# Probabilities times values per head in six spread slots, mirrored query order kept through the feed-forward, accumulators opened by transposes

## The reference

```
mask   = bucket(q @ proj) == bucket(k @ proj)          # 6 sign bits
attn   = softmax(where(mask, q @ k.T / 8, -1e9))       # 768 x 768 for each of 16 heads
x      = attn @ v, heads side by side                   # 2 x 768 x 512
u      = x + real(fft(fft(x, axis=seq), axis=feature))
ch     = relu(normalise(u) @ w_ch1) @ w_ch2             # 512 -> 2048 -> 512
x2     = u + ch
out    = (sigmoid(conv5(x2)) * (x2 @ w_val)) @ w_out
```

## Time and profile before

| | |
|---|---|
| median of the runs (3) | 663.28 us |
| the profiled execution | 663.62 us |
| its span (first to last instruction) | 661.8 us |
| PE busy / PEld busy | 634.2 us (96%) / 508.4 us (77%) |
| DVE, ACT, POOL busy | 353.8, 317.0, 245.4 us |
| chain that ended last: PE, DVE | 84%, 8% |
| granted TensorE clock | full in all of the 40 slices |

### The profile page before, as it was taken

One profiled execution on the slowest core, in us unless ns is written; L12 is line 12 of the kernel. 1 busy time (PEld: TensorE's weight loads), 2 busy tenths in 40 slices (PEclk: granted clock), 3 DMA queues, 4 the chain that ended last, 5 costly groups with the idle time before them and its releaser, 6 DMA issues.

```text
span 661.8 us, 11290 instructions
## 1 busy us (share of the span) xinstructions
PE 634.2 (96%) x3810; PEld 508.4 (77%) x3810; DVE 353.8 (53%) x585; ACT 317.0 (48%) x606; POOL 245.4 (37%) x201
## 2 busy tenths in 40 slices
PE   2999999999999999889999999999999999999998
PEld 1667676767666675888888888889888888888786
DVE  2978786968787785987211111115433333329920
ACT  2877776868686765364322222224333333255242
POOL 6643333333252440845333222235544444313140
PEclk9999999999999999999999999999999999999999
DMA  5922231314241000100122222431212222000102
GB/s 127 247 77 72 72 95 48 95 48 108 59 119 57 15 25 1 49 0 1 33 65 63 63 63 63 141 115 33 63 63 63 63 63 63 16 1 1 64 32 95
DMA packets 34263, 42.08 MB, mean 64 GB/s; under 512 B 3521, under 2 KB 22209, under 8 KB 34241
## 3 DMA queue, kind: packets, MB, share of 16 engines
q1 hardware_dynamic: 32512, 37.77, 19.7%
q0 software_dynamic: 1728, 4.02, 2.3%
HBM read 38.63 MB, written 3.15 MB: 63 GB/s over the span
## 4 chain that ended last, share of the span: by engine, by line
PE 84%; DVE 8%; issue 3%; POOL 2%; ACT 1%; DMA 1%; SPq 0%; DVEq 0%; ACTq 0%
PE banks L1516 20%; PE banks L1504 20%; PE banks L1319 10%; PE banks L1302 10%; PE banks L1366 7%; PE banks L1595 4%; PE banks L1611 4%; DVE row_min L970 2%; PE banks L1258 2%; PE banks L1439 2%; PE banks L1491 1%; DVE probT L342 1%; DVE k_b L963 1%; PE banks L1342 1%; POOL row_sums_and_differences L540 1%
## 5 line engine op out<-in xcount | busy, mean ns | idle before, releaser
L1165 DVE SCALAR_TENSOR_TENSOR h_lo<-banks,h_hi 128x512 fp32r<-128x512 f32 x64 | 35.5, 558 | 186.4 <-ACT h_hi L826 186.4
L970 DVE TENSOR_REDUCE row_min<-banks 128x1 f32<-128x768 f32 x96 | 91.3, 956 | 44.3 <-PE banks L1302 43.8
L677 ACT ACTIVATE prob<-banks,row_min 128x768 f32<-128x768 f32 x96 | 87.0, 906 | 30.1 <-DVE row_min L970 30.1
L1504 PE MATMUL banks<-unT_hi,w_hi 128*128 128x512 f32 (+1 forms) x256 | 86.5, 338 | 0.0
L1504 PE MATMUL banks<-unT_hi,w_lo 128*128 128x512 f32 (+1 forms) x256 | 86.3, 337 | 0.0
L1504 PE MATMUL banks<-unT_lo,w_hi 128*128 128x512 f32 (+1 forms) x256 | 86.2, 337 | 0.0
L1366 PE MATMUL banks<-ident,prob 128*128 128x128 f32 x576 | 79.7, 274 | 2.2 <-DVE probT L342 1.2
L563 POOL TENSOR_TENSOR w_lo<-w_stage,w_hi 128x512 fp32r<-128x512 f32 x32 | 45.1, 1411 | 83.2 <-ACT w_hi L742 83.2
L1366 PEld LDWEIGHTS banks<-ident,prob 128*128 128x128 f32 x576 | 67.2, 140 | 10.2 <-ACT probT L342 2.6
L501 POOL TENSOR_TENSOR k_b<-k_raw,k_a 64x768 fp32r<-64x768 f32 x16 | 29.2, 1823 | 123.2 <-ACT k_a L660 123.2
L1319 PE MATMUL banks<-probT,v_in 128*64 128x384 f32 x384 | 72.3, 498 | 0.7 <-ACT outT L687 0.7
(11 more groups left out here) (149 smaller groups left out, 1204.1 us busy)
## 6 DMA issues: line engine op xcount, KB each, us to landing
w_stage<-in_moe_w_ch SPq DMA_DIRECT2D x64, 256.0 KB, 2.8
q_raw<-in_q SPq DMA_DIRECT2D x32, 192.0 KB, 3.3
k_raw<-in_k SPq DMA_DIRECT2D x32, 192.0 KB, 3.6
v_in<-in_v SPq DMA_DIRECT2D x16, 192.0 KB, 2.4
out<-y_out SPq DMA_DIRECT2D x12, 256.0 KB, 2.0
seq_tables_sb<-in_dft POOLq DMA_DIRECT2D x6, 386.0 KB, 3.6
wvo_stage<-in_moe_w_val SPq DMA_DIRECT2D x1, 1024.0 KB, 5.4
wvo_stage<-in_moe_w_out SPq DMA_DIRECT2D x1, 1024.0 KB, 7.9
```

The costliest lines, as they stand in the source:

```text
L677: act.activation(prob[s % 2][:, :, :], s_tile(s), ACT.Exp, bias=row_min[:, s:s + 1], scale=-1.0, accum_out=row_sum[:, s:s + 1]).then_inc(e ...
L970: dve.tensor_reduce(row_min[:, s:s + 1], s_tile(s), AX.XY, ALU.min).then_inc(min_ready, 1)
L1165: dve.scalar_tensor_tensor(out=h_lo[:, slot, at:at + size], in0=h_bank[c], scalar=0.0, in1=h_hi[:, slot, at:at + size].bitcast(F32), op0=A ...
L1504: op = pe.matmul(h_bank[c], w_[:, slot, kb, :], x_[:, kb, at:at + size], start=(kb == 0 and m == 0), stop=(kb == KB - 1 and m == 2))
```

## The change

1. **Probabilities times values.** A group of products is now one head h with all 768 queries: the query half g = 0 in partitions 0 to 63 of bank 7, g = 1 in 64 to 127. There are still 24 matmuls a pair, in six groups of four, but the groups stand in slots 9, 11 (of the same pair), 1, 3, 5, 7 (of the next). `copy_outT` moves from slots 1 and 4 to 2 and 8, task O from slots 3 and 6 to 5 and 11, B from slots 1 and 7 to 0 and 6; C0 and C1 keep slots 2, 8 and 4, 10. The row sums are inverted per head, `write_x` writes 64 columns of six tiles instead of 128 columns of three. Since products now reach back further, pair 1 is written out and the loop runs over pairs 2 to 6.
2. **Row order.** `un_hi` and `un_lo` keep the folded order; `reverse` and `natural` are gone. `take_x2` restores the natural order while it drains, with one more instruction per block d (four instead of three, one of them a single column).
3. **Opening the accumulators.** `open_acc` issues one PE transpose for each of six tiles and each d: 24 a batch instead of 32 matmuls.
4. **Loads.** The values of each head have a semaphore and a load of their own; head 1's waits until the products of head 1 of the pair before are done.

```
-        PREPARE = {1: ["B"], 2: ["C0"], 4: ["C1"], 7: ["B"], 8: ["C0"], 10: ["C1"]}
+        PREPARE = {0: ["B"], 2: ["C0"], 4: ["C1"], 6: ["B"], 8: ["C0"], 10: ["C1"]}
-        OUT_SLOT = {3: 0, 6: 1}
+        OUT_SLOT = {5: 0, 11: 1}
-        PV_SLOTS = {11: (0, 0), 0: (0, 1), 1: (0, 2), 2: (1, 0), 3: (1, 1), 4: (1, 2)}
+        PV_SLOTS = {9: (0, 0, 0), 11: (0, 0, 1), 1: (1, 0, 2), 3: (1, 1, 0), 5: (1, 1, 1), 7: (1, 1, 2)}
...
-            def load_v(i):
-                need(sp, pv_done, 2 * i)
-                for h in range(2):
-                    sp.dma_start(v_in[:, h, :, :], v_v[2 * i + h]).then_inc(v_loaded, 16)
+            def load_v(i, h):
+                need(sp, pv_done, 2 * i + (h - 1) if not isinstance(i, int) or i else 0)
+                sp.dma_start(v_in[:, h, :, :], v_v[2 * i + h]).then_inc(v_loaded[h], 16)
...
-                    if s == 1 and not (isinstance(i, int) and i == 0):
+                    if s == 2 and not (isinstance(i, int) and i == 0):
                         copy_outT(i, 0)
-                    if s == 4 and not (isinstance(i, int) and i == 0):
+                    if s == 8 and not (isinstance(i, int) and i == 0):
                         copy_outT(i, 1)
...
-                    act.copy(half[:, 0:C0 - HALF], PS[:, d, HALF:C0]).then_inc(x2_by_act, 1)
-                    act.copy(half[:, C0 - HALF:HALF], acc(d, 1)).then_inc(x2_by_act, 1)
+                    act.copy(half[:, 0:1], PS[:, d, HALF:HALF + 1]).then_inc(x2_by_act, 1)
+                    act.copy(half[:, C1 + 1:HALF], PS[:, d, C0 - 1:HALF:-1]).then_inc(x2_by_act, 1)
+                    act.copy(half[:, C1:0:-1], acc(d, 1)).then_inc(x2_by_act, 1)
...
-                for kt in (2 * part, 2 * part + 1):
-                    for h in range(2):
-                        op = pe.matmul(PS[h * D:(h + 1) * D, 7, 0:HALF], v_in[:, h, kt, :],
+                for kt in range(T // PV_PARTS * part, T // PV_PARTS * (part + 1)):
+                    for g in range(2):
+                        op = pe.matmul(PS[g * D:(g + 1) * D, 7, 0:HALF], v_in[:, h, kt, :],
                                        probT[h][:, kt, g * HALF:(g + 1) * HALF], start=(kt == 0), stop=(kt == T - 1))
...
+                tiles = (range(C0 // P), range(C0 // P, T))[c]
+                for t in tiles:
+                    at = t * P - c * C0
+                    pe.matmul(acc(d, c)[:, at:at + P], X[:, b, t, d * P:(d + 1) * P], ident[:, :], is_transpose=True,
+                              start=(t == tiles[0] and (c == 0 or d % 2 == 0)), stop=False, skip_group_check=True)
```

More of the change, by code:

```diff
@@ L335, in drain_prob @@
             wait_filled(eng, i, use)
-            if h == 0 and qt % HT == 0:
-                need(eng, pv_done, pair_ * 2 + (qt // HT - 1))
+            if qt == 0:
+                need(eng, pv_done, pair_ * 2 + (h - 1))
             half = int(task[1])
@@ L428, in _ @@
             load_qk(0, 1)
-            load_v(0)
+            load_v(0, 0)
+            load_v(0, 1)
             load_qk(1, 0)
@@ L481, in _ @@
             pool.memset(ident[:, :], 0.0).then_inc(consts_ready, 1)
[L482 to L485, removed]
+            pool.wait_ge(consts_ready, 6)
             pool.affine_select(out=ident[:, :], in_=ident[:, :], compare_op=ALU.not_equal, fill=1.0,
@@ L732, in _ @@
             pair(0, 0)
-            with act.Fori(1, NP - 1) as i:
+            pair(1, 0)
+            with act.Fori(2, NP - 1) as i:
                 pair(i, 0)
@@ L757, in unT_hi @@
                 src = PS[:, un_bank(n), :].rearrange("p (k m) -> p k m", k=KB)
-                for rows, cols in natural(t):
-                    act.copy(un_hi[b][:, :, cols], src[:, :, rows]).then_inc(unT_hi_done, 1)
+                act.copy(un_hi[b][:, :, t * P:(t + 1) * P], src).then_inc(unT_hi_done, 1)
             def normalise(n):
@@ L1036, in pair @@
                             prepare(i, use)
-                    if s == 10 and last < 2:
+                    if s == 8 and last < 2:
                         invert_sums(i, 0)
-                    if s == 1 and not first:
+                    if s == 2 and not first:
                         invert_sums(i - 1, 1)
@@ L1044, in _ @@
             pair(0, 0)
-            with dve.Fori(1, NP - 1) as i:
+            pair(1, 0)
+            with dve.Fori(2, NP - 1) as i:
                 pair(i, 0)
@@ L1378, in pair @@
                     if s in PV_SLOTS:
-                        g, part = PV_SLOTS[s]
-                        if s == SLOTS - 1:
-                            if last < 2:
-                                p_times_v(i, g, part)
-                        elif not first:
-                            p_times_v(i - 1, g, part)
-            pe.wait_ge(consts_ready, 9)
+                        back, h, part = PV_SLOTS[s]
+                        if not back and last < 2:
+                            p_times_v(i, h, part)
+                        if back and not first:
+                            p_times_v(i - 1, h, part)
+            pe.wait_ge(consts_ready, 7)
             pe.wait_ge(w_ready, 2)
@@ L1391, in _ @@
             pair(0, 0)
-            with pe.Fori(1, NP - 1) as i:
+            pair(1, 0)
+            with pe.Fori(2, NP - 1) as i:
                 pair(i, 0)
@@ L1410, in transpose_un @@
                 if before is not None:
-                    pe.wait_ge(unT_lo_done, unT_pieces(before))
+                    pe.wait_ge(unT_lo_done, before + 1)
                 for kb in range(KB):
```

151 lines of the change are left out of this document (63 added, 88 removed).

## The result

| | before | after |
|---|---|---|
| median of the runs | 663.22 us (5 runs, 663.13 to 665.55) | 669.33 us (5 runs, 668.85 to 670.48) |
| the profiled execution, its span | 663.62, 661.8 us | 669.33, 667.6 us |
| slots 0 to 0 of the next pair, in the loop | 30.69 us | 32.03 us |
| batch 1's openings | 7.06 us | 2.96 us |

The changed kernel takes 1.0084 times as long (95% interval 1.0067 to 1.0101). By the medians it is 6.1 us slower, by the ratio 5.6 us; 667.6 had been predicted.

The account below looks back on a forecast made before the run. PE was taken to bound the kernel, with about 1.4 us of waiting per attention pair. Attention +9.5, openings -4.1 and -1.4, small edits +0.3 and -0.2 made +4.1 on 663.62 us: 667.6 forecast, range 658.5 to 671.5.

Parts of the forecast that it names:

- small edits: Behind attention: take_x2's extra copies +0.3 us, unfolding gone from the row drains -0.2; reverse, inverted sums, write_x and written-out pair 0.
- Slots: Attention loop, slot by slot: half a pair 5.35 + 4.96 + 5.72 us, pair 32.06 against 30.69, six pairs +8.2.
- The prediction's other way of counting: Attention pair: 1.4 us of exponential waits gone, 2.64 of new waits in, B's entry of 0.2 paid twice.
- Next late: What would wait next: O or products up to 0.25 us more each; after batch 1's openings, hidden-layer drains 0 to 0.5.
- Pair 0: First attention pair, with neither O nor a copy: slots 9 to 11 take about 7.5 us, +0.4 (0 to +0.9).
- Last pair and tail: Last pair and rest of attention up to the last fold: 42.8 us against 41.95, +0.9 (-1 to +2).
- Openings: Feed-forward accumulators opened by transposes: batch 1 from 7.06 to 3.0 us, -4.1; batch 0 -1.4 (-1.7 to -0.5).
- the rival of slow transposes: Accumulator openings: transposes run at half clock, so the openings give 3 + 1 us less, 671.6 us; chance 0.04.
- O was not in time: Rival in slots 5 and 11: C1's drain is in time, 14 waits of 0.88 us go, 655.3 us; chance 0.12.
- neither was the copy: Rival in slots 3 and 9: only outT's copy is in time, 14 waits of 0.44 us go, 661.4 us; chance 0.16.
- the loads were: Rival: head 1's q and k loads come late behind load_v, 2 us beyond the slack costing 14, 682 us; chance 0.05.
- the halves run side by side: Rival in attention products: the two halves run one after the other, 48 groups costing 1.44 us more each, 737; chance 0.03.

Follow-up runs that it names:

- B behind products: Changed kernel with products before O, outT copy before the exponential, sums inverted in slots 7 and 1, B moved to slots 1 and 7: 654.70 us, ratio 0.9850.
- sums late: The kernel with B behind products, but in pairs 0 and 7 the inversion of head 0's sums stays in slot 8: 651.64 us, ratio 0.9794 to before.
- the sums earlier: Changed kernel with products before O, outT copied before the exponential, and row sums inverted in slots 7 and 1 instead of 8 and 2: 657.64 us, ratio 0.9899.
- products before O: Changed kernel with only PE's order turned in slots 5 and 11, the group of products issued before task O: 659.46 us, ratio 0.9917 to before.
- copy before the exponential: Changed kernel with only ACT's order turned in slots 2 and 8, outT copied before the slot's exponential: 663.97 us, ratio 0.9991 to before.
- parts 2 and 3 alone: Kernel before with attention untouched and only the row order, take_x2 and transposed openings of the change: 658.53 us, ratio 0.9902 to before.
- the openings doubled: Changed kernel with batch 0's openings of the first column piece each issued twice, adding 16 transposes: 669.80 us, ratio 1.0080 to before.

## Why the prediction was right, step by step

The sign and the mechanism were right, and the time was 1.7 us short. The errors partly cancel: attention cost 1.4 us more than said and the openings gave 0.8 us less, while the small edits came out 0.5 us better.

*Slots.* 5.35, 4.96 and 5.72 were predicted; 5.34, 4.95 and 5.68 (5.76 in slots 10 and 11) were measured, the pair 32.03 us for 32.06, the six pairs +8.1 for +8.2. Both waits stand on the instructions named, with the releasers named, and each was taken away by itself for about its own price: 11.1 us by the ratios, 9.9 by the medians, for thirteen times 0.88 (11.4), and 6.2 or 5.4 us for the copy. The prediction's other way of counting, 2.64 of new waits and twice 0.2 for B against 1.4 of waits gone, gives 1.64 and not its 1.37; the sum over the slots was the better one. Its rivals counted 14 such waits, where the trace has 13: slot 11 of pair 7 has no C1 before it.

*Next late.* For the wait at O the sum held. For the copy it named nothing that follows; the exponential did, at 0.2 to 0.3 us in slots 4 and 10. It made no difference to the forecast, but it is why the two gains did not add.

*Pair 0.* +0.4 was said, within 0 to 0.9; +1.05 was measured, outside these bounds. Slots 9 to 11 take 7.91 (3.38, 1.46, 3.07) instead of 7.5, since the transposes of slot 9 start late behind its scores and the products queue behind them; the rest lies in slots 2 to 5. Pair 0 also differs between executions of the same code (25.99 and 26.84 in two kernels with equal attention), so a part of this may be no property of the change.

*Last pair and tail.* 42.8 us was said, 43.53 measured. The term left out is ACT's rounding of the folded parts, which the change had moved behind the copy; put back ahead of it, the stretch takes 42.78. The step counted the copies and the products, and not what stood behind the copy on ACT's queue.

*Openings.* Batch 1: -4.1 said and measured, at 0.12 us for each transpose and at a granted clock of 1.00 (450 to 475 above), so for these the rival of slow transposes is out; 0.18 us of the 2.96 is the wait for the first block's `h_lo`, given 0 to 0.5. Batch 0: -1.4 said, -1.21 where the clock stays full, -0.57 in the profiled execution: the term was sized at a clock that this stretch does not always have. So the rival of slow transposes came true in a part of batch 0's openings, for about 0.6 us of the 1 it had named. The prediction had argued against it from attention, where scores and products stand between the transposes; that could say little of a stretch without them.

*Small edits.* +0.3 and -0.2 us said, -0.3 and -0.15 measured behind and ahead of the openings. That is too small to be taken apart.

*Rivals.* O was not in time, and neither was the copy; the loads were; products cost 1.44 for four as before, so the halves run side by side. The advice of the Trainium skill ("Perfetto Trace Analysis", Optimization Strategy) to interleave regimes came out in the end: spread products, with the two waits removed, the sums inverted earlier and B moved back, beat every other kernel here (29.06 us a pair against 30.69). The spreading was good, and its places for O, the copy, the inversion and B were not. Whether the old layout would gain as much from the same care was not tried.

## What to carry to other kernels

Before a task is moved in a loop whose engines run in order, ask who had its buffer last and how many instructions of PE stand between that drain's start and the next user: the wait of 0.88 was covered or bare by the order of two neighbours in one slot. Remove waits one at a time, then look for what comes next; here six small edits, most of them read from the trace of the kernel before them, turned a loss of 0.8% into a gain of 2.3%. A change made of parts should be timed in parts: half of this one was worth 6 us by itself.

## What the runs showed of the hardware

**A tiny operation on DVE waits for a long one on POOL.** `row_den`, 128 x 6 elements from SBUF to SBUF, takes 0.16 us alone, and beside a POOL operation 1.84 us (pair 0 of the kernel with B behind products), 4.43 us (its pair 7) and 1.44 us (sums late). Each time it ends within 0.1 us of POOL's. In the kernel with the sums earlier it is so in every pair of the loop, with 1.58 to 1.74 us beside `q_a`. The rows of pair 0:

```profile
31.70 1.84 POOL L492 TENSOR_TENSOR q_a<-q_raw,q_a 64x768 fp32r<-64x768 f32 x1
31.73 1.84 DVE L963 TENSOR_SCALAR row_den<-row_sum 128x6 f32<-128x6 f32 x1
```

Beside the folds of pair 7, DVE's copies and reductions out of PSUM keep their 0.55 and 0.96 us. The Trainium skill ("SBUF — State Buffer", "SBUF: two separate sides") describes an exclusive lock on ports that DVE and GpSimd share, held for a whole instruction; the trace agrees, at 4.43 us. In the longest case its record begins during the first fold (234.03) and ends behind the second (238.46), so a second POOL operation went ahead of it.

**The granted clock falls now and then, most often in batch 0's openings.** In seventeen runs of the kernel before, the five with a mean clock of 1.000 took 662.8 to 663.3 us, and the nine with 0.997 took 664.7 to 665.6: nearly 2 us more. Its one trace shows no fall, so where those nine had theirs is not known. Eleven traces have each of batch 0's openings once, as transposes. In eight of them, the changed kernel's among them, the clock fell to 0.50 within these openings, where PE runs only transposes with pauses between. With the openings doubled it did not fall. Four traces show falls behind other pauses, two of them only there. These are rows of busy time (columns as in the earlier trace rows), in this order: products before O, before and in its fall; copy before the exponential, the same place without a fall; parts 2 and 3 alone, at its fall; B behind products, at its fall behind the wait for `row_den`.

```profile
312.00:314.00 2.00, 1.05 (x10) 0.81 (x9) 1.66 (x6) 1.30 (x2) 0.97 (x2) 1.00 0.00 0
314.00:316.00 2.00, 0.86 (x8) 0.62 (x7) 1.16 (x5) 1.08 (x2) 1.20 (x4) 1.00 0.00 0
316.00:318.00 2.00, 2.00 (x12) 1.61 (x10) 1.27 (x2) 1.39 (x3) 0.00 (x0) 0.58 0.00 0
...
316.00:318.00 2.00, 1.05 (x9) 0.81 (x9) 1.53 (x5) 1.30 (x2) 1.26 (x2) 1.00 0.00 0
318.00:320.00 2.00, 0.94 (x8) 0.70 (x7) 1.30 (x7) 0.79 (x2) 1.20 (x4) 1.00 0.00 0
320.00:322.00 2.00, 1.72 (x12) 1.27 (x12) 1.11 (x3) 1.69 (x4) 0.00 (x0) 1.00 0.00 0
...
294.00:296.00 2.00, 0.39 (x3) 0.42 (x4) 1.34 (x6) 2.00 (x7) 0.55 (x1) 1.00 0.00 0
296.00:298.00 2.00, 2.00 (x12) 1.95 (x11) 2.00 (x7) 1.05 (x2) 0.00 (x0) 0.64 0.00 0
...
236.00:240.00 4.00, 1.34 (x10) 1.07 (x8) 3.97 (x5) 1.31 (x3) 2.67 (x3) 1.00 0.12 40
240.00:242.00 2.00, 1.96 (x9) 1.00 (x11) 1.71 (x2) 2.00 (x6) 0.00 (x0) 0.68 0.00 0
```

The first two kernels have the same work and the same pauses in this place, and only one of them has the fall. What decides it is open. In batch 1, 24 transposes in a row behind a busy stretch ran at 1.00, so there the rule of the Trainium skill that transposes don't count for the clock ("TensorE: Matmul & The Clock Gate", Part 4) cost nothing. In batch 0's openings such a rule and the pauses would show alike; the doubled transposes, with which the clock stayed full, speak against the rule, and the fall at 240 followed a pause behind ordinary matmuls. No run here has these pauses with ordinary matmuls in the transposes' place.
